# Linear attention's numerators one slot later, TensorE's slot in another order, full tiles as two column halves of 64

## The reference

```python
def phi(x):
    proj = np.einsum('bhsd,df->bhsf', x, w_phi)
    proj = proj - np.max(np.abs(proj), axis=-1, keepdims=True)
    return np.concatenate([np.exp(proj), np.exp(-proj)], axis=-1)
q_p, k_p = (phi(q), phi(k))
kv = np.einsum('bhsf,bhsd->bhfd', k_p, v)
z = np.sum(k_p, axis=2)
num = np.einsum('bhsf,bhfd->bhsd', q_p, kv)
den = np.einsum('bhsf,bhf->bhs', q_p, z)[..., None] + 1e-06
attention = num / den
...
e_idx = np.argmax(x @ w_gate, axis=1)      # one expert a row
out[mask] = gate_w * eom * (np.maximum(x[mask] @ w1[e], 0.0) @ w2[e])
...
g = xn @ w_gate; silu = g / (1.0 + np.exp(-g))
result = silu * (xn @ w_val) @ w_out
```

## Time and profile before

| what | value |
|---|---|
| time, median of 3 runs | 910.85 us (910.55 to 911.68) |
| time of the profiled execution | 910.34 us |
| its span in the profile | 908.7 us |
| TensorE busy | 886.8 us, 98% |
| VectorE busy | 432.3 us, 48% |
| ScalarE busy | 293.9 us, 32% |
| attention, until the first product with expert weights | 224.33 us of the span |

### The profile page before, as it was taken

The page is one execution under the profiler, slowest core; times in us unless marked ns, Lnnn a source line. Parts: engine busy times, 40 slices in busy tenths (PEclk is TensorE's granted clock), DMA queues, the critical chain, the costliest instruction groups (busy, mean ns, idle before and its releaser), DMA issues.

```text
span 908.7 us, 15622 instructions
## 1 busy us (share of the span) xinstructions
PE 886.8 (98%) x5888; PEld 811.7 (89%) x5889; DVE 432.3 (48%) x875; ACT 293.9 (32%) x479; POOL 123.4 (14%) x145
## 2 busy tenths in 40 slices
PE   8999999999999999999999999999999999999996
PEld 6795968779999999999988999999999999999996
DVE  5678687898767644333457422222222222222222
ACT  4545454572155532223353321121112112112111
POOL 1010302122344112222300010010001001001001
PEclk9999999999999999999999999999999999999999
DMA  9513713112457432346743630030020002000000
GB/s 296 178 54 124 271 52 104 53 48 59 157 177 196 79 58 71 26 78 122 159 157 114 181 112 1 1 105 1 0 70 35 0 2 102 0 0 35 1 1 35
DMA packets 37181, 75.31 MB, mean 83 GB/s; under 512 B 8176, under 2 KB 24688, under 8 KB 35472
## 3 DMA queue, kind: packets, MB, share of 16 engines
q1 hardware_dynamic: 32832, 56.07, 23.2%
q0 software_dynamic: 3488, 17.85, 5.3%
q10 hardware_dynamic: 816, 0.79, 0.3%
HBM read 51.06 MB, written 23.64 MB: 82 GB/s over the span
## 4 chain that ended last, share of the span: by engine, by line
PE 89%; DVE 5%; issue 2%; ACT 2%; DMA 1%; POOL 0%; POOLq 0%; DVEq 0%; SPq 0%; ACTq 0%
PE ps L1023 10%; PE ps L1025 10%; PE ps L1024 10%; PE ps L822 6%; PE ps L1038 5%; PE ps L1039 5%; PE ps L1037 5%; PE ps L925 4%; PE ps L938 3%; PE ps L926 3%; PE ps L927 3%; PE ps L940 3%; PE ps L939 3%; PE ps L769 3%; PE ps L729 2%
## 5 line engine op out<-in xcount | busy, mean ns | idle before, releaser
L1023 PE MATMUL ps<-xnH,blkH 128*128 128x384 f32 x576 | 193.7, 336 | 3.0 <-DVE blkL L1690 1.9
L1025 PE MATMUL ps<-xnH,blkL 128*128 128x384 f32 x576 | 193.4, 336 | 0.0
L1024 PE MATMUL ps<-xnL,blkH 128*128 128x384 f32 x576 | 193.2, 335 | 0.0
L1697 DVE TENSOR_TENSOR sg<-sg,ps 128x384 f32<-128x384 f32 x72 | 39.8, 553 | 245.5 <-ACT sg L1256 241.6
L1256 ACT ACTIVATE sg<-ps 128x384 f32<-128x384 f32 x72 | 35.4, 491 | 252.1 <-PE ps L1025 252.1
L1023 PEld LDWEIGHTS ps<-xnH,blkH 128*128 128x128 f32 x576 | 108.2, 188 | 7.5 <-issue 4.3
L1024 PEld LDWEIGHTS ps<-xnL,blkH 128*128 128x128 f32 x576 | 108.2, 188 | 2.6
L1025 PEld LDWEIGHTS ps<-xnH,blkL 128*128 128x128 f32 x576 | 108.1, 188 | 0.0
L1038 PE MATMUL ps<-blkL,hH 128*128 128x512 f32 x216 | 84.8, 393 | 0.0
L1039 PE MATMUL ps<-blkH,hL 128*128 128x512 f32 x216 | 84.8, 392 | 0.0
L1037 PE MATMUL ps<-blkH,hH 128*128 128x512 f32 x216 | 84.5, 391 | 0.0
(11 more groups left out here) (219 smaller groups left out, 1593.6 us busy)
## 6 DMA issues: line engine op xcount, KB each, us to landing
stage<-in_ffn_w SPq DMA_DIRECT2D x12, 768.0 KB, 4.3
xin<-xs_dram SPq DMA_DIRECT2D x9, 578.2 KB, 9.9
xs_dram<-zrow SPq DMA_DIRECT2D x8, 578.2 KB, 8.6
qT<-in_q SPq DMA_DIRECT2D x4, 1152.0 KB, 5.5
xnH_dram<-xoH SPq DMA_DIRECT2D x8, 576.0 KB, 3.5
xnL_dram<-xoL SPq DMA_DIRECT2D x8, 576.0 KB, 6.1
xnH<-xnH_dram SPq DMA_DIRECT2D x6, 768.0 KB, 5.4
xnL<-xnL_dram SPq DMA_DIRECT2D x6, 768.0 KB, 6.3
```

Of the source, the lines that this page charges most:

```text
L1023: e.matmul(o, hi, xnH[par][:, c, :], start=(c == 0), stop=False)
L1024: e.matmul(o, hi, xnL[par][:, c, :], start=False, stop=False)
L1025: last = e.matmul(o, lo, xnH[par][:, c, :], start=False, stop=(c == KC - 1))
```

## The change

The numerators of a query tile move on TensorE from slot t+2 to slot t+3, and the division on VectorE from t+3 to t+4. In a slot TensorE now does: first half of numerators, first half of projections, second half of numerators, then key sums, transposes, second half of projections. Each numerator matmul of a full tile becomes two, for 64 positions (columns of the stationary operand) each, as those of packed tiles are already; so do four small matmuls in `turn`. A packed tile's numerators go to bank 2, which the transposes use, and with that one wait in `key_sums` falls away and one ahead of the first transposes of a batch comes in. The pieces of expert weights on VectorE move to other slots, two of them to slot 8. Behind batch 3 the expert rows' first transposes come between the numerators of tiles 7 and 8.

```diff
         def num_of(at):
 
-            first = KVB if at[1] % NJ % 2 == 1 else ZB
+            first = 2 if packed(at) else KVB if at[1] % NJ % 2 == 1 else ZB
             return ps[:, first:first + 2, 0:4 * VA].rearrange("p b (h e) -> p b h e", e=VA)
...
-        split_slots_dve = [(B - 1, sl) for sl in (1, 2, 5, 6, 7, 8, 9)] + [(B, 0)]
+        split_slots_dve = [(B - 1, sl) for sl in (2, 4, 5, 7, 8, 8, 9)] + [(B, 0)]
...
-        XT_FIRST = (2, 3, 1, 0)
+        XT_FIRST = (3, 1, 0, 2)
...
-                if j == 0 and not first:
-                    e.wait_ge(s["dve_N"], at[0] * NJ)
-                    settle(e, "carry_pe")
                 for c in range(KC):
                     last = e.matmul(ps[c * 32:(c + 1) * 32, ZB, :], ones[0:n, 0:32], ex[0:n, buf, :, 2 * c:2 * c + 2, :],
...
                         for i in range(4):
-                            last = e.matmul(ps[:, TURNED[1], ZC + i * KC:ZC + (i + 1) * KC], zT[:, i, :], zsel[:, :],
-                                            start=True, stop=True)
+                            for g in range(2):
+                                last = e.matmul(ps[rows_half(g), TURNED[1], ZC + i * KC:ZC + (i + 1) * KC],
+                                                zT[:, i, rows_half(g)], zsel[:, :], start=True, stop=True)
...
-                    elif at[1] > NJ + 1:
+                    elif at[1] > NJ + 1 and not packed(at):
                         e.wait_ge(s["dve_N"], nkq((at[0], at[1] - 2)))
...
                 for h in range(half * 4, half * 4 + 4):
                     for sign in range(2):
-                        last = e.matmul(num_of(at)[0:n, h // 4, h % 4, :], ex[:, at[1] % 2, sign, h, 0:n],
-                                        kvs[:, h // 2, sign * 2 + h % 2, :], start=(sign == 0), stop=(sign == 1))
+                        for g in range(2):
+                            last = e.matmul(num_of(at)[rows_half(g), h // 4, h % 4, :],
+                                            ex[:, at[1] % 2, sign, h, rows_half(g)],
+                                            kvs[:, h // 2, sign * 2 + h % 2, :], start=(sign == 0), stop=(sign == 1))
...
             def slot(b, sl):
 
-                g1, g2 = (before_slot(b, sl, n) for n in (1, 2))
+                g1, g2, g3 = (before_slot(b, sl, n) for n in (1, 2, 3))
                 first_batch = isinstance(b, int) and b == 0
-                turned = sl == NJ + 2 and has_slot(b)
-                if turned:
+                short = is_q(g3) and packed(g3)
+                if sl == NJ + 2 and has_slot(b):
                     turn(b)
+                if is_q(g3) and not short:
+                    numerators(g3, 0)
                 if has_slot(b):
                     projections(b, sl, 0)
+                if short:
+                    numerators(g3, 0)
+                if is_q(g3):
+                    numerators(g3, 1)
+                if short and has_slot(b):
+                    projections(b, sl, 1)
                 if is_k(g2):
                     key_sums(g2)
                 if is_q(g1):
...
                     elif not (isinstance(g1[0], int) and g1[0] == 0):
                         e.wait_ge(s["act_Q"], g1[0] * NJ)
+                        e.wait_ge(s["dve_N"], g1[0] * NJ)
+                        settle(e, "carry_pe")
...
-                if is_q(g2) and not turned:
-                    numerators(g2, 0)
-                if has_slot(b):
+                if has_slot(b) and not short:
                     projections(b, sl, 1)
-                if turned:
-                    numerators(g2, 0)
-                if is_q(g2):
-                    numerators(g2, 1)
...
             def first_transposes():
                 e.wait_ge(s["gt"], GS)
                 for c in range(KC):
+                    if c == KC - 1:
+                        e.wait_ge(s["act_Q"], B * NJ)
                     x_transpose(c, XT_FIRST[c])
...
             with e.If(early > 0):
-                e.wait_ge(s["act_Q"], B * NJ)
+                e.wait_ge(s["act_Q"], B * NJ - 1)
                 first_transposes()
             slot(B, 1)
             with e.If(early > 0):
                 e.wait_ge(s["dve_XT"], KC)
+            slot(B, 2)
+            with e.If(early > 0):
                 once(0, 0)
                 hidden(0, 0, 0)
                 hidden(0, 0, 1)
                 e.wait_ge(s["dve_N"], B * NJ)
                 hidden(0, 0, 2)
                 outputs(0, 0, 0)
-            for sl in range(2, TAIL_SLOTS):
+            for sl in range(3, TAIL_SLOTS):
                 slot(B, sl)
...
             def slot(b, sl):
-                g3 = before_slot(b, sl, 3)
+                g4 = before_slot(b, sl, 4)
                 if sl == NJ + 2 and has_slot(b):
                     turned_evac(b)
-                if is_q(g3):
-                    normalise(g3)
+                if is_q(g4):
+                    normalise(g4)
...
                 if isinstance(b, int) and (b, sl) in split_slots_dve:
-                    n = split_slots_dve.index((b, sl))
-                    split_low(n, 0, n + 1)
+                    for n, at in enumerate(split_slots_dve):
+                        if at == (b, sl):
+                            split_low(n, 0, n + 1)
```

## The result

The changed kernel takes 906.01 us (median of 4 runs, 905.33 to 906.86) beside 911.06 us for the kernel before (median of 4 runs). The ratio is 0.9949, 95% interval 0.9936 to 0.9963: 5.05 us faster, where 11.2 were forecast. The run that was profiled took 906.86 us, its span is 905.2.

What follows compares the result with a forecast made beforehand. TensorE, busy 98% of the span, was taken as the bound; gains of 3.6 + 3.6 + 3.9 + 0.1 = 11.2 us took the profiled 910.3 to 899.1, the median to 899.6 us. The range was 896 to 904.5.

Steps and rivals of the forecast that it cites:

- What the halves cost: Full tiles' numerators in attention: two half-width pieces of 1.29 us replace 3.49 us, leaving about 0.75 us gained a tile.
- What the later slot moves: Attention batches: evener TensorE slots cut waits from 1.3 to 0.7 us; distances fall by 3.6, 3.6 and 3.9 us.
- VectorE holds the batches: Rival, chance 0.14: VectorE's slots 9 to 3 carry 1 to 1.5 us more, gain a batch about 2.2, time 903.6.
- TensorE's own work is thus some 51.4 us a batch: Attention before the change: TensorE busy nearly throughout a batch, apart from short waits for VectorE's low parts.
- 48.5 + 0.7 = 49.2 us: A batch after the change: 49.2 us with 0.7 us of waits for VectorE, instead of 52.8.
- This stretch saves 0.1 us: From batch 3's tile 5 numerators to the first expert product: 22.67 us before, only 0.1 us saved, TensorE waiting about 4.
- the rival that the clock falls: Rival, chance 0.15: TensorE's clock drops after the new 4 us stall at attention's end, 2 to 5 us lost, 903.
- the third step of `hidden`: End of attention: 0.3 us for this step, which needs a low part VectorE makes behind two divisions and a routing step.
- All behind starts earlier by the sum: After the first expert product: VectorE's table and POOL's weight loads move along, so the whole gain of 11.2 us is kept.

Runs made afterwards that it cites:

- halves_old: The kernel before with only full tiles' numerators as two column halves, slots and order as before: 897.51 us, ratio 0.9871, beside 909.20 us before.
- whole_new: The changed kernel with full tiles' numerators as whole full-width matmuls again, so the new order alone: 913.97 us, ratio 1.0016.
- scatter_late: The changed kernel with POOL's scatter of a batch's rows held until behind slot 8 of the running batch: 915.32 us, ratio 1.0036.
- warm_tail: The changed kernel with 20 unused fp32 matmuls filling TensorE's idle ahead of the expert rows' first transposes: 898.39 us, ratio 0.9891.
- after_4: The changed kernel unchanged, run again on a fourth chip, where nothing stalled: 902.68 us, ratio 0.9894, beside 911.46 us before.
- v_late_2: The changed kernel with the next batch's v loaded after slot 8, repeated on a third chip: 907.24 us, ratio 0.9946.
- after_again: The changed kernel unchanged, run a second time on another chip, with stalls: 909.65 us, ratio 0.9979, beside 911.57 us before.
- v_late: The changed kernel with the load of the next batch's v held until slot 8's projections are done: 900.06 us, ratio 0.9900.
- warm_tail_2: The changed kernel with 20 unused matmuls ahead of the expert rows' first transposes, run once more: 898.96 us, ratio 0.9892.
- tile5_mixed: The changed kernel with tile 5's even heads as half-width and odd heads as full-width numerators: 904.31 us, ratio 0.9935.
- gate_first: The changed kernel with POOL looking at the early flag after one copied tile of batch 3 instead of two: 899.28 us, ratio 0.9889.
- tile5_whole_warm: The changed kernel with tile 5's numerators at full width and 20 unused matmuls ahead of the expert rows' first transposes: 907.18 us, ratio 0.9976.

## Why the prediction was off

**What the halves cost: right.** A piece takes 1.27 us (1.29 forecast).

**What the later slot moves: right for the undisturbed batch, a little mis-sized.** The wait at the start of slot 2, forecast at 0.7 us, is 0.83 (line 729, for `tL` of line 1333), and the undisturbed distances are 48.75, 48.76 and 49.2 instead of 49.2, 49.2 and 49.9: 4.1, 4.0 and 4.6 us less than the earlier trace rows, and not 3.6, 3.6 and 3.9. The rival that VectorE holds the batches falls. But most of this gain comes from the halves: they alone give 3.6, 3.5 and 3.8 us (halves_old), where the sum gave them 3.0. The order alone gives 1.5, 1.2 and 0.4 us (whole_new). The kernel before was profiled once, so differences between chips may be in both. That the forecast came near for the two together is thus partly luck: alone they would add up to 5.1, 4.7 and 4.2 us.

**The step that failed first: "TensorE's own work is thus some 51.4 us a batch", and a batch "takes 48.5 + 0.7 = 49.2 us".** The sum held no idle without a wait, because the trace before has none in attention. In the profiled run batches 1 and 2 took 50.42 and 51.56 us instead of the undisturbed 48.76 and 49.2: 1.66 + 2.34 = 4.0 us lost to stalls beside the scatter (batch 2's piece alone lost 3.63 - 1.27 = 2.36). That they go with the scatter is shown on one chip (scatter_late moved them with it). By what means the scatter holds TensorE up, why a kernel with short rows has stalls and one with long rows hasn't, why most batches 3 are spared, and why three comparisons show them and those on two other chips don't, stays open.

**"This stretch saves 0.1 us": wrong by 1.8 us, by the rival that the clock falls.** It takes 217.30 - 192.90 = 24.40 us, before 22.67, forecast 22.6. The mechanism was as told: 4.77 us of idle (about 4 forecast), ended by POOL, whose gating came behind its copy, which a division released. The copy began after 14.44 us (14.5 forecast), but the transposes after 18.2, where 17.2 were forecast: copy and look at the flag took 1.07 us instead of 0.65, and the gating with its hand-over 2.66 instead of 2.03, of which the gating itself is 2.52. The larger part is the clock: 0.64 us on the transposes and 0.97 on tile 8's numerators. The two are more than 1.8 together because the forecast carried some slack: its terms end at 22.1, or 22.4 with the third step of `hidden`, and it booked 22.6. `warm_tail`, which has the clock full, gains 1.6 us at that point. The forecast gave the rival 0.15, since the trace before had no idle stretch of this length. The Trainium skill, "TensorE: Matmul & The Clock Gate", section HAM oscillation, says that idle gaps between bursts of matmuls bring the half clock back; the trace agrees, with a granted clock of 0.53 behind 4.77 us of idle.

**"All behind starts earlier by the sum": wrong by 3.5 us in the profiled run.** Of 7.03 us at the first expert product 5.05 are left ahead of the dense layer, and 3.18 at the last sum of squares, 8 us later. In the first stretch 1.0 us goes ahead of the first sum of squares, where TensorE waits 0.82 us for a low part that VectorE makes late (line 931; forecast 0.3), and another 1.0 us by 300.71, behind the transfer of raw weights, 15.88 us long and now on the chain, where it waits 1.26 instead of 0.28 us. In the second, 1.88 us of idle was followed by the lower clock, where 1.57 us before was not. This comes and goes: at that place the clock fell behind 1.83 us of idle in `after_4` and 2.78 in `v_late_2`, and stayed full behind 1.90 in `after_again` and 2.25 in `scatter_late`; `v_late` and `warm_tail_2` idle under 1 us there.

**The sum.** 0.08 us gained at the start and 8.68 in the batches, less 1.73 in the tail and 3.53 behind, leave 3.5 us of the span. The profiled run was the longest of its four; the median gains 5.05. Without stalls the same kernel gains 8.8 us (after_4), and 9.1 with v late (v_late): forecast 11.2. So the stalls are more than half of what was missed, and the clock and what follows the tail the rest.

## What to carry to other kernels

A gain of TensorE's own time that is read from rows is real, but it buys idle stretches where another engine's chain ends last, and with a clock that falls behind idle such a stretch costs more than its length: fill it, or leave work where it covers part of that chain. A fill must be measured in the whole kernel, for one of the fills here made it 5.5 us slower at a place far behind. On both chips where the halves alone ran, they were at least as fast as the halves with the new order; each part of a change should be tried by itself. A stall that shows as "issue" in a stream of very short matmuls should be looked for on more than one chip before its cause is named.

## What was not expected of the hardware

- Streams of short rows stall beside GpSimd's scatter in three comparisons (the first, whose chip is not on record, and those on the second and third chip) and not on two other chips, with the same program: 0.18 to 1.12 us each, and 1.3 to 2.4 us a batch where the clock stayed full.
- Half-width rows of 64 columns take about the same whether the column half changes every matmul or every second one (1.27 and 1.33 us for 32 rows). The 36 ns a row are a mean: in the trace of the kernel after two rows start 6 ns apart and the next pair about 64 ns later, where full-width rows start 112 ns apart.
- A change between full-width and half-width fp32 rows costs some 0.15 us (tile5_mixed).
- POOL's gating of the expert rows takes 2.03 us before, 2.52 after and 3.07 in gate_first and halves_old, with the same three instructions.
- Once TensorE stood still for 5.1 us in the dense layer with no wait, beside a transfer at 384 GB/s (tile5_whole_warm). All ten runs of that kernel are long (905.28 to 908.37 us), beside 901.72 for the same kernel without the fill.
